# Splitting the first chunk of an attention-plus-two-MLP kernel into two half-width units

## What is computed

```python
def _attn_ref(q, k, v, alpha):          # B, H, S, D = 4, 8, 768, 48
    for t in range(S):
        state = alpha[:, :, t, :, None] * state + np.einsum('bhd,bhe->bhde', k[:, :, t], v[:, :, t])
        y[:, :, t] = np.einsum('bhd,bhde->bhe', q[:, :, t], state)

x = transpose(attn).reshape(3072, 384)
x = np.maximum(x @ w_in, 0.0) ** 2 @ w_out        # w_in 384x2048, w_out 2048x384
h = x @ w2_in
out = (h * (1.0 / (1.0 + np.exp(-h)))) @ w2_out
```

## Time and profile before

| | |
|---|---|
| median of 3 runs | 950.53 us (946.99 to 951.72) |
| the profiled execution | 952.14 us |
| its span | 950.5 us |
| TensorE matmuls busy | 916.7 us, 96% |
| VectorE, ScalarE, POOL busy | 449.2 us, 403.4 us, 81.2 us |
| mean granted TensorE clock | 0.989 |
| chain that ended last | PE 94%, VectorE 2%, issue 1%, DMA 1% |

### The profile page before, as it was taken

The page is one execution under the profiler, slowest core; times in us unless marked ns, Lnnn a source line. Parts: engine busy times, 40 slices in busy tenths (PEclk is TensorE's granted clock), DMA queues, the critical chain, the costliest instruction groups (busy, mean ns, idle before and its releaser), DMA issues.

```text
span 950.5 us, 12762 instructions
## 1 busy us (share of the span) xinstructions
PE 916.7 (96%) x4822; PEld 764.8 (80%) x4822; DVE 449.2 (47%) x684; ACT 403.4 (42%) x744; POOL 81.2 (9%) x119
## 2 busy tenths in 40 slices
PE   5668999999999999999999999999999999999997
PEld 5657888888888888888888888888888888888897
DVE  5578888667777766667334421221311312212310
ACT  3335455445444544454466653322333323333520
POOL 6633320000000000000013300000000000000000
PEclk9798999999999999999999999999999999999999
DMA  9834443422332342231033310110110100200100
GB/s 185 199 102 114 108 119 78 108 61 61 94 76 68 77 114 64 61 95 21 14 103 97 101 67 1 34 33 1 34 34 1 54 13 1 67 1 1 33 9 28
DMA packets 97235, 60.09 MB, mean 63 GB/s; under 512 B 55824, under 2 KB 87184, under 8 KB 97168
## 3 DMA queue, kind: packets, MB, share of 16 engines
q1 hardware_dynamic: 92928, 46.53, 20.0%
q0 software_dynamic: 4096, 12.59, 4.6%
q10 hardware_dynamic: 144, 0.10, 0.0%
HBM read 45.02 MB, written 9.44 MB: 57 GB/s over the span
## 4 chain that ended last, share of the span: by engine, by line
PE 94%; DVE 2%; issue 1%; DMA 1%; ACT 0%; SPq 0%; POOL 0%; DVEq 0%; POOLq 0%
PE h_ps L531 41%; PE z_ps L544 39%; PE job_ps L562 3%; PE job_ps L483 3%; PE job_ps L516 3%; PE job_ps L512 2%; PE job_ps L500 1%; PE job_ps L489 1%; PE z_ps L562 1%; DMA w_raw<-in_moe_w_out 1%; DVE rcp L841 1%; PE job_ps L455 0%; PE h_ps L568 0%; SPq L289 0%; DMA nat_a<-in_alpha 0%
## 5 line engine op out<-in xcount | busy, mean ns | idle before, releaser
L908 DVE TENSOR_TENSOR g_lo<-g,g_hi 128x512 fp32r<-128x512 f32 x177 | 124.2, 702 | 317.9 <-ACT g_hi L713 242.9
L531 PE MATMUL h_ps<-x_hi,win_hi 128*128 128x512 f32 x576 | 225.1, 391 | 7.9 <-ACT g L710 4.9
L531 PE MATMUL h_ps<-x_lo,win_hi 128*128 128x512 f32 x576 | 224.7, 390 | 0.0
L531 PE MATMUL h_ps<-x_hi,win_lo 128*128 128x512 f32 x576 | 224.6, 390 | 0.0
L708 ACT ACTIVATE g<-h_ps 128x512 f32<-128x512 f32 x96 | 57.5, 599 | 232.0 <-PE h_ps L531 232.0
L710 ACT ACTIVATE g<-h_ps 128x512 f32<-128x512 f32 x96 | 57.4, 598 | 199.3 <-PE h_ps L531 175.6
L531 PEld LDWEIGHTS h_ps<-x_hi,win_hi 128*128 128x128 f32 x576 | 108.5, 188 | 30.9 <-issue 8.4
L531 PEld LDWEIGHTS h_ps<-x_lo,win_hi 128*128 128x128 f32 x576 | 108.6, 189 | 22.6
L531 PEld LDWEIGHTS h_ps<-x_hi,win_lo 128*128 128x128 f32 x576 | 108.5, 188 | 22.6
L544 PE MATMUL z_ps<-g_hi,wout_hi 128*128 128x512 f32 x288 | 118.5, 411 | 0.0
L713 ACT ACTIVATE g_hi<-g 128x512 fp32r<-128x512 f32 x177 | 111.8, 632 | 5.6
(11 more groups left out here) (126 smaller groups left out, 938.4 us busy)
## 6 DMA issues: line engine op xcount, KB each, us to landing
w_raw<-in_moe_w_in POOLq DMA_DIRECT2D x32, 192.0 KB, 3.0
w_raw<-in_moe_w_out POOLq DMA_DIRECT2D x32, 192.0 KB, 3.1
v_sb<-in_v SPq DMA_DIRECT2D x48, 96.0 KB, 2.7
z_scratch<-z_sb SPq DMA_DIRECT2D x18, 256.0 KB, 2.5
x_raw<-z_scratch SPq DMA_DIRECT2D x6, 768.0 KB, 4.5
out_x<-z_sb SPq DMA_DIRECT2D x80, 48.0 KB, 1.7
nat_a<-in_alpha SPq DMA_DIRECT2D x40, 88.0 KB, 2.2
nat_k<-in_k SPq DMA_DIRECT2D x40, 88.0 KB, 2.2
```

The lines of the kernel that those rows point to most:

```text
L531: last = nc.tensor.matmul(h_ps[f % 2][:], w[:, f, tile(kk)], x[par][:, kk, :], start=(kk == 0 and n == 0), stop=(kk == KD - 1 and n == 2))
L908: nc.vector.tensor_tensor(low, g[f % 2][:], high.bitcast(F32), ALU.subtract).then_inc(g_lo_made, 1)
```

## The change

Chunk 0 becomes two units of 256 columns: unit 0 holds batches 0 and 1 of it, unit 1 batches 2 and 3. There are then 7 units of the first MLP (`UNITS1`), and the pairs are numbered `j`, 0 to 27: 0 to 3 are unit 0's, 4 to 7 unit 1's (both 256 columns), from 8 on 512 columns as before. Only pairs 0 to 3 lie ahead of the first product; pairs 4 to 7 lie beside unit 0's products, pairs 8 to 11 (chunk 1) beside unit 1's. TensorE turns a, k and q for pairs 0 to 7.

The first MLP's weights are loaded once, in four groups, into the place where their low parts will be (`win_raw`, `wout_raw`), with no ring; POOL waits for chunk 0's q before the first two groups. Chunk 0's inputs are loaded per batch by transfers of four or eight heads, those of batch 1 issued by ScalarE. The state of chunk 0 is written by one operation per head instead of a copy and a product. ScalarE squares the running products before the reciprocals are there, copies `kp_t` and `y` a pair later than before, and splits two chunks of weights in each of the pairs 2 and 3, four more before the last part of x, and then two per step.

```diff
+FIRST = 2
+UNITS1 = UNITS + 1
+WGROUPS = [(0, 2), (2, 6), (6, 11), (11, 16)]
-FIRST_PE = {0: 6, 1: 8, 2: 8, 3: 4}
-WARM_AFTER = 24
+EARLY = FIRST * PAIRS
+WARM_AFTER = 20
+EARLY_SPLITS = {2: 2, 3: 2}
+EARLY_CHUNKS = 8
+def batches(u):
+    return range(2 * u, 2 * u + 2) if isinstance(u, int) and u < FIRST else range(BATCH)
+def cols(u):
+    return slice(0, P * len(batches(u)))
-def stage_step(kind, n):
-    if n < 2 * PAIRS:
-        return {"A": -1, "KQ": 1, "S": 2, "I": 3, "Y": 3}[kind] + 3 * (n - PAIRS)
-    return {"A": -21, "KQ": -19, "S": -18, "I": -17, "Y": -16}[kind] + 4 * n
+def stage_step(kind, j):
+    u, p = divmod(j, PAIRS)
+    if u < FIRST:
+        return {"A": -1, "KQ": 1, "S": 2, "I": 3, "Y": 3}[kind] + 3 * p
+    return {"A": -21, "KQ": -19, "S": -18, "I": -17, "Y": -16}[kind] + NF * u + 4 * p
...
+            for i, (f0, f1) in enumerate(WGROUPS):
+                if i < 2:
+                    pool.wait_ge(nat_first_in["q"][i], 32)
+                for kk in range(KD):
+                    pool.dma_start(win_raw[:, f0:f1, tile(kk)],
+                                   w1_in[tile(kk), f0 * P:f1 * P].rearrange("p (f n) -> p f n", n=P)).then_inc(w1_arrived[0][i], 16)
+                pool.dma_start(wout_raw[:, f0:f1, :], w1_out[f0 * P:f1 * P, :].rearrange("(f p) d -> p f d", p=P)
+                               ).then_inc(w1_arrived[1][i], 16)
...
+            def a_stage(j):
+                if j < PAIRS:
+                    wait(pe, scanned, scans(j - 1))
+                else:
+                    wait(pe, kt_copied, j)
+                turn("a", j, a_bank(j)).then_inc(a_made, 1)
...
-                        last = nc.tensor.matmul(h_ps[f % 2][:], w[:, f, tile(kk)], x[par][:, kk, :],
+                        last = nc.tensor.matmul(h_ps[f % 2][:, x_cols(u)], w[:, f, tile(kk)], x[par][:, kk, x_cols(u)],
...
             for kind, n in AHEAD:
-                if kind == "S":
-                    keep_warm(FIRST_PE[n])
                 stage(kind, n)
+            pe.wait_ge(scanned, scans(PAIRS))
             keep_warm(WARM_AFTER)
...
-            for n in range(PAIRS):
-                bounds(n)
-                for c in range(5 * n, 5 * n + 3):
-                    split_chunk(c)
-                kt_copy(n)
-                for c in range(5 * n + 3, 5 * n + 5):
-                    split_chunk(c)
-                y_copy(n)
-            split_x(0, ys=1)
-            bounds(PAIRS)
+            for j in range(PAIRS):
+                bound_decay(j)
+                if j:
+                    kt_copy(j - 1)
+                bound_reciprocal(j)
+                if j:
+                    y_copy(j - 1)
+                for _ in range(EARLY_SPLITS.get(j, 0)):
+                    split_chunk(done)
+                    done += 1
+            kt_copy(PAIRS - 1)
+            split_x(0, 0, ys=1, tiles=[0])
+            y_copy(PAIRS - 1)
+            split_x(0, 0, ys=1, tiles=[1])
+            for n in range(done, EARLY_CHUNKS):
+                split_chunk(n)
+            split_x(0, 0, ys=1, tiles=[2])
+            bound_decay(PAIRS)
+            bound_reciprocal(PAIRS)
...
+                if u < FIRST:
+                    for n in (EARLY_CHUNKS + 2 * F, EARLY_CHUNKS + 2 * F + 1):
+                        if n < NCHUNK:
+                            split_chunk(n)
...
-                last = nc.vector.tensor_copy(inc[r], own)
+                nc.vector.tensor_tensor(state[r, p, bs, r], sums(j, h, 2), decay_end[r, p, bs].unsqueeze(2).to_broadcast([HD, 2, HD]),
+                                        ALU.mult).then_inc(state_made, 1)
```

More of the change, by code:

```diff
@@ new lines, in load_nat @@
+            def load_nat(kind, j):
+                wait(sp, {"a": a_made, "k": k_made, "q": q_made}[kind], max(EARLY, j - 1))
+                wait(sp, filled, FILLED)
+                u, p = divmod(j, PAIRS)
+                for q4 in range(QUADS):
+                    rows = qkva[kind][:, 2 * p + q4 // 2].rearrange("b (s c) d -> s b (c d)", c=GROUP)[bass.ts(u - 1, P // GROUP)]
+                    first, last = (32, GROUP * HD) if q4 % 2 else (0, (GROUP - 1) * HD + 32)
+                    sp.dma_start(by_four[kind][j % 2][32 * q4:32 * (q4 + 1), :, 0:last - first], rows[:, :, first:last]
+                                 ).then_inc(nat_in[kind][j % 2], 16)
@@ new lines, in load_v, with repack, stage @@
+            def load_v(j):
+                wait(sp, y_made, j - 1 if j >= EARLY + 2 else 0)
+                load_pair("v", j // PAIRS - 1, j % PAIRS, v_sb[j % 2][:], v_in[j % 2])
+            def repack(p, at=slice(0, UT)):
+                for row, kk, to, n in repack_pieces(p):
+                    sp.dma_start(x_raw[to:to + n, kk, at], y_sb[p % 2][row:row + n, at]).then_inc(y_moved[p % 2], 16)
+            def stage(kind, j):
+                more = EARLY <= j + 2 < JOBS
+                ahead = {EARLY - 1: [EARLY, EARLY + 1]}.get(j, [j + 2] if EARLY <= j and more else [])
+                if kind == "A" and j == PAIRS - 1:
+                    load_second("a")
+                if kind == "KQ" and j == PAIRS - 1:
+                    load_second("k")
+                    load_second("q")
+                if kind == "A":
+                    for n in ahead:
+                        load_nat("a", n)
+                if kind == "KQ":
+                    for n in ahead:
+                        load_nat("k", n)
+                        load_nat("q", n)
@@ new lines, in kq_stage, with s_stage @@
+            def kq_stage(j):
+                if j < PAIRS:
+                    wait(pe, q_scaled, j)
+                else:
+                    wait(pe, scanned, scans(j + 1))
+                turn("k", j, k_bank(j)).then_inc(k_made, 1)
+                if j == PAIRS:
+                    wait(pe, masked, 2 * j - 1)
+                if j > PAIRS:
+                    wait_i_taken(pe, j - 1)
+                turn("q", j, q_bank(j)).then_inc(q_made, 1)
+            def s_stage(j):
+                wait(pe, k_scaled, j + 1)
+                wait(pe, q_scaled, j + 1)
+                wait(pe, y_copied, j)
+                if j > EARLY and has_state(j - 1):
+                    wait_i_taken(pe, j - 1)
+                nb = len(batches(j // PAIRS))
+                for b in range(nb):
@@ new lines, in i_stage, with y_stage @@
+            def i_stage(j):
+                wait(pe, kt_copied, j + 1)
+                wait_v(pe, j)
+                if j >= PAIRS:
+                    wait(pe, masked, 2 * j + 1)
+                for b, v2 in enumerate(v_of(j)):
+                    last = nc.tensor.matmul(i_bank(j)[0:ROWS, b * 2 * HD:(b + 1) * 2 * HD], kp_t[:, b, :], v2,
+                                            start=True, stop=True)
+                last.then_inc(i_made, 1)
+            def y_stage(j):
+                wait_v(pe, j)
+                wait(pe, masked, 2 * (j + 1))
+                ps, p = job_ps[2], j % PAIRS
+                if j >= EARLY:
+                    before = state_before(j)
+                    wait(pe, state_made, 2 * (before + 1))
+                    for b in range(BATCH):
+                        nc.tensor.matmul(ps[0:ROWS, tile(b)], state[:, p, b, :], qp[j % 2][:, tile(b)],
@@ L730, in _ @@
             act.wait_ge(table_loaded, 1)
[L731 to L748 removed]
+            done = 0
@@ L871, in i_stage @@
+            def i_stage(j):
+                wait(dve, i_made, j + 1)
                 for h in (0, 1):
                     r = head_rows(h)
[L873 to L878 removed]
```

624 lines of the change are left out of this document (316 added, 308 removed).

## The result

| | before | changed kernel |
|---|---|---|
| median | 951.1 us (946.99 to 952.6, 4 runs beside it) | 983.8 us (982.0 to 984.6, 4 runs) |
| ratio | | 1.0348, 95% interval 1.0312 to 1.0384 |
| span of the profiled execution | 950.5 | 981.3 |
| mean granted clock | 0.989 | 0.973 |
| mark (start of step 2's product) | 72.12 | 52.66 |

The changed kernel is 3.5% slower. The sign is that of the prediction, but the size is not: 958 was expected, with a range to 968. The sum had a span of 958.1. The measured one is 23.2 longer: 17.5 at the start (a gain of 19.5 instead of 37; against the mark of 35, which is rounded, 17.7) and 5.7 behind the mark (50.3 more than before where 44.6 were expected). The execution is also 3.3 us longer than its span, where it was 1.6 before; no run looked into this difference of 1.6.

The account below looks back on a forecast made before the run. The prediction took TensorE's work, plus what it loses before 84 us, as the bound. Its terms, -37 + 17.8 - 2 + 4.2 + 18.6 + 6 = +7.6, gave a median of 958 us, range 934 to 968.

Parts of the forecast that it names:

- The start: Before step 2's product: shorter pairs and ScalarE's new order bring that instant from 72.12 to 35, a gain of 37 us.
- Rival 4: At the start: loads hold it, sixteen large weight transfers sharing the engines; 5 us more, 963 us; chance 0.05.
- TensorE's additional work: After the mark: more, shorter product instructions (+5.9) and attention of pairs 4 to 7 (+11.9), together +17.8 us.
- the old disturbance: Just after the mark: 5.0 us lost to half clock and a wait becomes 3, so -2 us.
- kt_copy: Unit 0: TensorE waits for ScalarE's `kp_t` copy before transposing `a` of pairs 5 to 7, 1.4 each, +4.2 us.
- VectorE's chain: Unit 1: VectorE's ordered work on 512-column pairs makes TensorE wait ahead of scores, cycles of 16.8, +18.6 us.
- rival 1: Unit 1: VectorE's chain does not hold TensorE, the start's gain survives; 934 us; chance 0.25.
- The clock: Unit 1: granted clock falls behind five waits, 1.2 us each, +6 us; ends 0 and 17.
- Rival 2: Unit 1: the loop is right, but the clock stays up between the waits; 952 us; chance 0.15.
- rival 3: Unit 1: clock falls and stays low through nearly the whole part that counts, 16 instead of 6; 968 us; chance 0.13.

Follow-up runs that it names:

- run 1: Changed kernel with the third and fourth groups of first weights issued later by POOL: 973.0 us.
- run 7: Changed kernel with only the fourth group of first weights issued later, the third sent at once: 977.2 us.
- Run 3: Changed kernel with 14 small matmuls whose result nobody needs ahead of the scores of pairs 8 to 12, inside the waits: 972.5 us.
- Run 4: Kernel before with only the change's reordering of ScalarE's early work, without the two units: 940.3 us.
- run 9: Changed kernel with two weight groups late, scans of pairs 8 to 12 a step earlier, and ScalarE's squares of pair 4 behind step 0: 959.8 us.
- run 10: Kernel before with ScalarE's new early order, and its squares of pair 4 behind step 1's activations: 936.0 us.

## Why the prediction was wrong, point by point

**The start (-37; measured -19.5): the step that failed.** The pairs' time was nearly right (22.1 against 21.0), so the halved VectorE work was well read from the rows. Wrong was the term for the loads: nothing in the sum, and 5 in the bound ("40 if the loads, of which all the first weights now stand in the queues at once, come 5 late"). I took the loads as a small disturbance of a known chain. But what the first part of x needs, pair 1's repack, goes through SyncE's queue, and the changed stream of TensorE also puts the turning of pair 4's `a`, a load that x does not need, ahead of pair 3's increment and `y`. Runs 1 and 7 show that GpSimd's weights held both up, in proportion to their bytes. I had not added up their bytes: 6.29 MB against 312 GB/s is 20 us. To turn pair 4's `a` later would not have been enough: ScalarE had the first part of x only at 38.78, and pair 3's `y` is copied behind it. At 40.37 that copy started some 1.2 after the part was done, which is my estimate of all that this could gain; no run tried it. Rival 4 had the mechanism of the transfers ("POOL issues sixteen large weight transfers at once") with 5 us and a chance of 0.05. The size was 11.3 by run 1 (52.66 - 41.41). The other 6.4 are the increment and the turning ahead of `y`, the half clock there and the four weight splits (run 1), which the sum left out; together 17.7. The mark also lies behind 42, which the prediction had named as a sign of being wrong.

**TensorE's additional work (+17.8): right, as far as shown.** The 0.120 per 256-column product stands in the trace. A short pair costs TensorE 3.0 where the sum had 3.2: from one turning of `a` to the next (70.52 to 81.29) are 10.77, of which 1.31 is the wait and 54 products are 6.48. What is left over from the sum behind the mark, once the waits and the clock below are set apart, is -1.0; it holds this term and the -2 for the old disturbance, which was not measured by itself. The columns/2.4 plus 2.5 ns that the prediction sets beside its rows is, by the Trainium skill ("TensorE: Matmul & The Clock Gate", section "Back-to-back issue gap"), the gap of an isolated matmul and not of a stream of weight loads and matmuls, as this kernel has. The rows decided here either way (0.227 and 0.120).

**kt_copy (+4.2; measured 4.9).** Right: 2.29 (the profile puts this one down to the low half before it, but the copy of `kp_t`, 57.70 to 58.04, ended last) and twice 1.31. The prediction's own parts add up to 2.32 and not the 2.4 that it went on with, so to waits of 1.3.

**VectorE's chain (+18.6; measured 19.2).** Right, and with it rival 1 is out: none of the waits was hidden. The first took 4.48 (3.7 in the sum), the four behind it 3.47 to 3.48 (3.5), pair 13's 0.79 (0.9). Run 3 shows the cycle of 16.8 by itself.

**The clock (+6; measured 11.4): the second miss.** The mechanism was right, the term too small. I took 1.2 per wait, about a third of the 3.4 that was its upper end; it was 2.3, with the clock at 0.50, the level of the earlier trace rows, for 3.4 to 6.8 us behind each of the five long waits (0.71, 0.50, 0.50 and 0.58 in the windows of 2 us from 102 to 110). Rival 2, the clock staying up, is out. The bounds (0 and 17) held it; rival 3's 16 was about as near as the 6.

**The chances.** Slower was right. The range ended at rival 3's 968 because I let one rival at a time happen. Start and clock are independent losses of the same sign, and both came: 958 + 17.7 + 5.7 (5.4 of it the clock's) + 1.6 outside the span = 983.

**What of the change pays.** Run 4 says that ScalarE's order alone is worth 10.8 us. With that order in both, the two units with weights in place, at their best here (run 9), stand 23.8 above run 10. The mark is 13.0 earlier (39.77 against 52.81), but from there it takes 35.0 more (916.7 against 881.7). By my sum 17.8 of this is TensorE's additional work; run 9's waits are 18.6 (8.1 + 6.0 + 4.5) against 5.0 in run 10; the 3.6 left go with the clock, a mean of 0.985 against 0.996, and were not tried apart. The time outside the span adds 1.4; the last 0.4 lie between the profiled executions and the medians. Units and weights in place were not tried apart, so how the 23.8 splits between them stays open.

## What to carry to other kernels

When a change sends bulk transfers at the start, add up their bytes against the time there is, and hold back those that nothing early needs: here they delayed the loads, and also the issue of small transfers on another engine's queue. A load that a reordered stream makes early is a gate for all that stands behind it. Halving a tile's columns about halves TensorE's time per product (0.227 to 0.120) but not the vector work beside it; where the slack was 1.5 us in 21, VectorE's chain became the bound, and the granted clock fell behind the waits. Idle products pay only while there is idle time for them: they were worth 11.3 us with the waits in place and cost 5.4 once the waits were gone.

## What the hardware showed that I had not expected

- The issue of three small transfers on SyncE's queue itself took 14.27 us while GpSimd's large ones were under way (9.24 and 3.97 with fewer of them), so the whole queue behind it stood, not only the transfer.
- A wait of 3.5 us in an 18 us cycle, TensorE otherwise busy, was enough each time for the granted clock to go to 0.50, the 1.2 GHz level; each cost 2.3 us on top. With shorter waits it went either way: in run 9 the clock fell behind waits of 1.94 (at 124.51) and 1.93 (at 155.02), and stayed at 1.00 behind one of 2.74 (at 109.37).
- The changed kernels' executions are 3.0 to 3.5 us longer than their spans, those of the kernel before and its variants 1.6 to 1.7; no run was made on the cause.
